# Experts with more than 256 rows: inner rows of three tiles at once instead of two tiles and one more

## The reference, cut to what matters

```python
logits = x @ w_gate                       # 1536 rows, 384 wide, 8 experts
expert_idx = np.argmax(logits, axis=1)
# each expert keeps up to capacity = 384 rows, in order: disp[e]
h = np.maximum(np.einsum('ecd,edf->ecf', disp, w1), 0.0)   # inner rows, 1024 wide
y = np.einsum('ecf,efd->ecd', h, w2)                       # outputs, 384 wide
out[i] = gate_w[i] * y[expert_idx[i], pos[i]]
```

## Time and profile before

| | us |
|---|---|
| median of 3 runs | 458.02 (458.01 to 459.62) |
| the profiled execution | 458.81 |
| its span, first to last instruction | 457.1 |
| VectorE busy | 309.7 (68%) |
| ScalarE busy | 255.3 (56%) |
| GpSimd busy | 57.8 (13%) |

### The profile page before, as it was taken

One profiled execution on the slowest core, in us unless ns is written; L12 is line 12 of the kernel. 1 busy time (PEld: TensorE's weight loads), 2 busy tenths in 40 slices (PEclk: granted clock), 3 DMA queues, 4 the chain that ended last, 5 costly groups with the idle time before them and its releaser, 6 DMA issues.

```text
span 457.1 us, 14532 instructions
## 1 busy us (share of the span) xinstructions
PE 431.2 (94%) x5882; PEld 409.5 (90%) x5882; DVE 309.7 (68%) x763; ACT 255.3 (56%) x527; POOL 57.8 (13%) x78
## 2 busy tenths in 40 slices
PE   2789999999999999999999999999999999999994
PEld 2678899999999999999999999998997789999994
DVE  4787966757686769677867737558556877678510
ACT  2164866456645654565545566575448876686421
POOL 7300000000000100001000200221020333321201
PEclk9999999999999999999999999999999999999998
DMA  8717795880130015001000157431966998610001
GB/s 275 274 60 238 261 325 183 284 329 4 49 145 4 2 44 185 3 1 39 3 1 3 40 209 275 142 120 27 315 215 208 313 353 275 206 61 0 32 1 44
DMA packets 35642, 63.39 MB, mean 139 GB/s; under 512 B 3980, under 2 KB 21950, under 8 KB 35568
## 3 DMA queue, kind: packets, MB, share of 16 engines
q1 hardware_dynamic: 33264, 57.88, 37.3%
q0 software_dynamic: 2304, 4.47, 2.6%
HBM read 50.77 MB, written 14.19 MB: 142 GB/s over the span
## 4 chain that ended last, share of the span: by engine, by line
PE 82%; DVE 6%; issue 5%; ACT 2%; DMA 2%; POOL 1%; POOLq 0%; SPq 0%; DVEq 0%; ACTq 0%
PE bank L718 21%; PE bank L704 19%; PE pair L625 6%; PE bank L931 6%; PE bank L884 5%; PE pair L586 3%; PE pair L884 3%; PE pair L899 3%; PE bank L938 3%; PE bank L899 3%; DVE AD L1224 2%; PE pair L644 2%; DVE KS L1215 2%; DMA stage<-in_moe_w_in 2%; PE pair L679 1%
## 5 line engine op out<-in xcount | busy, mean ns | idle before, releaser
L704 PE MATMUL bank<-XH,W 128*128 128x256 f32 x576 | 118.6, 283 | 0.9 <-ACT RB L1073 0.9
L718 PE MATMUL bank<-W,GH 128*128 128x384 f32 x372 | 98.4, 345 | 0.0
L704 PEld LDWEIGHTS bank<-XH,W 128*128 128x128 f32 x576 | 94.9, 189 | 1.9 <-issue 1.2
L704 PE MATMUL bank<-XL,W 128*128 128x256 f32 x288 | 80.6, 280 | 0.0
L718 PEld LDWEIGHTS bank<-W,GH 128*128 128x128 f32 x372 | 61.7, 188 | 1.3
L1073 ACT ACTIVATE RB<-bank 128x256 f32<-128x256 f32 x96 | 36.7, 382 | 46.6 <-PE bank L704 45.9
L718 PE MATMUL bank<-W,GL 128*128 128x384 f32 x186 | 62.6, 337 | 0.0
L1276 DVE TENSOR_TENSOR GL<-GG,GH 128x256 fp32r<-128x256 f32 x96 | 40.6, 423 | 32.0 <-ACT GH L970 31.5
L970 ACT ACTIVATE GH<-GG 128x256 fp32r<-128x256 f32 x96 | 40.1, 418 | 35.9 <-PE bank L718 34.4
L1215 DVE TENSOR_TENSOR KS<-KS 128x512 f32<-128x512 f32 x72 | 50.3, 699 | 8.8 <-PE pair L625 8.8
L704 PEld LDWEIGHTS bank<-XL,W 128*128 128x128 f32 x288 | 54.3, 188 | 0.0
(11 more groups left out here) (165 smaller groups left out, 716.5 us busy)
## 6 DMA issues: line engine op xcount, KB each, us to landing
raw<-in_moe_w SPq DMA_DIRECT2D x23, 768.0 KB, 7.5
stage<-in_moe_w SPq DMA_DIRECT2D x9, 768.0 KB, 8.1
KS<-in_krw SPq DMA_DIRECT2D x12, 512.0 KB, 5.9
slots<-X SPq DMA_DIRECT2D x8, 579.0 KB, 6.6
VV<-in_v SPq DMA_DIRECT2D x12, 288.0 KB, 6.9
KS<-in_krw SPq DMA_DIRECT2D x12, 256.0 KB, 6.1
stage<-in_moe_w_in SPq DMA_DIRECT2D x4, 768.0 KB, 7.0
stage<-in_moe_w_out SPq DMA_DIRECT2D x4, 768.0 KB, 7.2
```

What stands on the lines that cost most here:

```text
L704: last = nc.tensor.matmul(bank[4 + f % 2][:, 0:2 * P], win[wa][:, c, f * P:(f + 1) * P], xa[:, c, :], start=n == 0, stop=n == 3 * KM - 1)
L718: last = nc.tensor.matmul(bank[6 + m][:, 0:DM], ga[(NF * g + f) % G3][:, cols], wout[wa][:, f, :], start=f == 0 and n == 0, stop=f == NF - ...
```

## The change

Experts with more than 256 rows no longer take the small way for their third tile. `hidden2` gets the number of tiles, and the branches choose between a copy of it that moves 384 columns and one that moves 256; both copies stand in the program. ACT's and DVE's counterparts read 384 or 256 columns the same way. The small way stays for experts of up to 128 rows alone. The three semaphores of the third tile go. On PE:

```diff
-            def hidden2(e):
+            def hidden2(e, tiles):
                 if e > 0:
-                    pe.wait_ge(xl2_ready, MT * e + 2)
+                    pe.wait_ge(xl2_ready, MT * e + tiles)
...
-                            last = nc.tensor.matmul(bank[HB[f % 3]][:, 0:2 * P], w1s(e, wa)[:, c, f * P:(f + 1) * P],
-                                                    xa[:, c, 0:2 * P], start=n == 0, stop=n == 3 * KM - 1)
+                            last = nc.tensor.matmul(bank[HB[f % 3]][:, 0:tiles * P], w1s(e, wa)[:, c, f * P:(f + 1) * P],
+                                                    xa[:, c, 0:tiles * P], start=n == 0, stop=n == 3 * KM - 1)
...
             for e in range(NE):
                 rows = pe.value_load(count_u[0:1, e:e + 1])
                 with pe.If(rows <= P):
-                    hidden_small(e, 0, h2_done)
-                    pe.sem_inc(h3_done, NFE)
+                    hidden_small(e)
                 with pe.Else():
-                    hidden2(e)
                     with pe.If(rows > 2 * P):
-                        hidden_small(e, 2, h3_done)
+                        hidden2(e, MT)
                     with pe.Else():
-                        rows_in(e + 1, 0)
-                        pe.sem_inc(hs_done, 2)
-                        pe.sem_inc(h3_done, NFE)
+                        hidden2(e, 2)
+                    rows_in(e + 1, 0)
+                    pe.sem_inc(hs_done, 2)
                 rows_in(e + 1, 1)
                 outputs2(e, 0)
```

`outputs2` loses its waits on hh3_ready and hl3_ready. On ACT (DVE is alike, with `hidden_low`):

```diff
-            def hidden_high(e):
+            def hidden_high(e, tiles):
                 for f in range(NFE):
                     act.wait_ge(h2_done, NFE * e + f + 1)
-                    nc.scalar.activation(HH[:, f, 0:2 * P], bank[HB[f % 3]][:, 0:2 * P], ACT.Relu).then_inc(hh_ready, 1)
+                    nc.scalar.activation(HH[:, f, 0:tiles * P], bank[HB[f % 3]][:, 0:tiles * P],
+                                         ACT.Relu).then_inc(hh_ready, 1)
...
                 with act.Else():
-                    hidden_high(e)
                     with act.If(rows > 2 * P):
-                        hidden_high_small(e, 2, h3_done, hh3_ready)
+                        hidden_high(e, MT)
                     with act.Else():
-                        act.sem_inc(rh_ready, 2)
-                        act.sem_inc(hh3_ready, NFE)
+                        hidden_high(e, 2)
+                    act.sem_inc(rh_ready, 2)
```

More of the change, by code:

```diff
@@ L146, in rwkv_moe_kernel @@
         SB = (5, 2)
-        SMALL = {0: (2, 4), 2: (7, 3)}
+        SMALL = (2, 4)
         XB = (0, 1, 4)
@@ L898, in hidden_small @@
                         for wa, xa in ((0, XH2), (0, XL2), (1, XH2)):
-                            last = nc.tensor.matmul(bank[SMALL[m][c]][:, 0:CF], xa[:, k_, m * P:(m + 1) * P],
+                            last = nc.tensor.matmul(bank[SMALL[c]][:, 0:CF], xa[:, k_, 0:P],
                                                     w1s(e, wa)[:, k_, c * CF:(c + 1) * CF],
@@ L907, in hidden_small @@
                     pe.wait_ge(rh_ready, 2 * e + c + 1)
-                    if m == MT - 1:
-                        pe.wait_ge(hl_ready, NFE * (e + 1))
                     for f in range(NFE // 2):
@@ L912, in hidden_small @@
                                                    RH[:, c * NFE // 2 + f, :], ident[:, :])
-                    last.then_inc(done, NFE // 2)
+                    last.then_inc(h2_done, NFE // 2)
             def outputs2(e, m):
@@ L1108, in _, with hidden_high_small @@
                 first_rows_high(q)
-            def hidden_high(e):
+            def hidden_high(e, tiles):
                 for f in range(NFE):
                     act.wait_ge(h2_done, NFE * e + f + 1)
-                    nc.scalar.activation(HH[:, f, 0:2 * P], bank[HB[f % 3]][:, 0:2 * P], ACT.Relu).then_inc(hh_ready, 1)
+                    nc.scalar.activation(HH[:, f, 0:tiles * P], bank[HB[f % 3]][:, 0:tiles * P],
+                                         ACT.Relu).then_inc(hh_ready, 1)
                     if f == 2 and e > 0:
                         split_high_expert(e, CH - 1)
-            def hidden_high_small(e, m, done, ready):
-                if m == 0 and e > 0:
+            def hidden_high_small(e):
+                if e > 0:
                     split_high_expert(e, CH - 1)
@@ L1123, in hidden_high_small @@
                     copy(RH[:, c * NFE // 2:(c + 1) * NFE // 2, :],
-                         bank[SMALL[m][c]][:, 0:CF].rearrange("p (f n) -> p f n", n=P)).then_inc(rh_ready, 1)
+                         bank[SMALL[c]][:, 0:CF].rearrange("p (f n) -> p f n", n=P)).then_inc(rh_ready, 1)
                 for c in range(2):
-                    act.wait_ge(done, NFE * e + (c + 1) * NFE // 2)
-                    nc.scalar.activation(HH[:, c * NFE // 2:(c + 1) * NFE // 2, m * P:(m + 1) * P],
+                    act.wait_ge(h2_done, NFE * e + (c + 1) * NFE // 2)
+                    nc.scalar.activation(HH[:, c * NFE // 2:(c + 1) * NFE // 2, 0:P],
                                          bank[SB[c]][:, :].rearrange("p (f n) -> p f n", n=P),
-                                         ACT.Relu).then_inc(ready, NFE // 2)
+                                         ACT.Relu).then_inc(hh_ready, NFE // 2)
             def weighted(e, m):
@@ L1502, in hidden_low, with hidden_low_small @@
                         split_low_expert(e, CH - 1)
[L1504 to L1507, removed]
+            def hidden_low_small(e):
+                for x in (CH - 2, CH - 1):
+                    split_low_expert(e, x)
                 for c in range(2):
-                    dve.wait_ge(high, NFE * e + (c + 1) * NFE // 2)
+                    dve.wait_ge(hh_ready, NFE * e + (c + 1) * NFE // 2)
                     fs = slice(c * NFE // 2, (c + 1) * NFE // 2)
-                    nc.vector.scalar_tensor_tensor(out=HL[:, fs, m * P:(m + 1) * P],
+                    nc.vector.scalar_tensor_tensor(out=HL[:, fs, 0:P],
                                                    in0=bank[SB[c]][:, :].rearrange("p (f n) -> p f n", n=P), scalar=0.0,
-                                                   in1=HH[:, fs, m * P:(m + 1) * P].bitcast(F32), op0=ALU.max,
-                                                   op1=ALU.subtract).then_inc(ready, NFE // 2)
+                                                   in1=HH[:, fs, 0:P].bitcast(F32), op0=ALU.max,
+                                                   op1=ALU.subtract).then_inc(hl_ready, NFE // 2)
             for e in range(NE):
```

26 lines of the change are left out of this document (9 added, 17 removed).

## The result

The changed kernel takes **460.6 us** (median of 20 runs, 457.87 to 463.35) against 458.49 for the kernel before on the same chip: ratio 1.0048, 95% interval 1.0029 to 1.0067. It is slower, as predicted, but by 2.1 us and not by 7.1. Its profiled execution took 460.7 us, with a span of 459.0 us.

What follows compares the result with a forecast made beforehand. TensorE (PE), busy 431.2 of 457.1 us, was taken as the bound. Code waits of +9.9 and PE's work of -2.8 gave +7.1, from the 458.02 median to 465.1 us; range 457.5 to 470.

Steps and rivals of the forecast that it cites:

- PE's own work: Experts 0 and 7: third tile's small way removed, wider matmuls added; -1.4 us each, -2.8 together.
- Evictions cost nothing: ScalarE and DVE reading 384 columns at once is covered by PE's work: cost 0; rival that they bind: 457.2, chance 0.04.
- waits for code: PE waiting for 256-instruction program blocks after taken branches: sum of code +9.9 us; forecast of slower by code, chance 0.62.
- Expert 3: Its jump to block 48 adds +1.0 us, and L956 (later L947) into block 49 adds +0.8.
- Expert 6: Its 256-column code lies in block 54, right behind the jump into block 53: +1.6 us.
- expert 1's skip: Jump from block 42 to 44 over block 43, the only one asked for: +5.3 us; alone passes the 2.8 deciding the sign.
- its clock: Expert 1's pause of 5 us drops PE's granted clock to 0.50: +1.0 us, between nothing and 3.5.
- entering a block asks for the next one: Rule for PE's program blocks, only two held; a block takes 3.7 us idle and about 6 us busy.
- Expert 2: Jump from block 45 to 46 +0.3 us; block 47 asked for at the join, pause 0.7 for 1.71, -1.0.
- Expert 4: 256-column code starts 16 instructions ahead of block 50: wait of 1.8 to 4.1 us, taken as +2.0.
- The rival of blocks at the idle price: Experts' stage leaves DMA freer, so blocks arrive at the idle price: +2.9 less 2.8, 458.1 us; chance 0.12.

Runs made afterwards that it cites:

- the pair without branches: Kernel before and changed kernel, each with arms chosen at build time from this input's counts: 454.06 us (ratio 0.9911) and 452.34 (0.9861).
- The padded kernel before: Kernel before with 82 never-executed PE instruction slots added per expert, giving the changed kernel's 544: 460.22 us, ratio 1.0034.
- the branchless one: Changed kernel with its arms chosen at build time from this input's counts, without branches: 452.34 us, ratio 0.9861.
- moved 40 ahead: Changed kernel with PAGE_PAD 128 for 160, so expert 1's jump stands 40 instructions ahead of block 43: 472.29 us, ratio 1.0294.
- moved 72 ahead: Changed kernel with PAGE_PAD 96 and a never-taken branch in expert 1; its jump stands 72 ahead of block 43: 467.38 us, ratio 1.0194.
- four other layouts of the changed kernel's arms: Changed kernel with copies swapped at PAGE_PAD 128 and 224 (466.43, 459.36 us), and with small path last at 160 and 112 (466.81, 463.75).
- PAGE_PAD 128: 128 instead of 160 semaphore increments on PE ahead of the experts: changed kernel 472.29 us, changed kernel with swapped copies 466.43.
- the kernel with 24: Changed kernel with PAGE_PAD 144 for 160, so expert 1's jump stands 24 instructions ahead of block 43: 461.91 us, ratio 1.0065.
- swapped: Changed kernel with the 256-column copy of hidden2 ahead of the 384-column one: 457.0 us, ratio 0.9960.

## Why the prediction was right and wrong

**Right: PE's own work.** The 384-column rows took 12.50 us for 72 matmuls in expert 7 (427.96 to 440.46), against 8.64 and 5.38 of small way: -1.52, predicted -1.4; in all -1.57 and -1.60 where -1.4 and -1.4 were said. Evictions cost nothing in the experts' stage, as argued; the pair without branches shows it.

**Right: waits for code, not the change's computation, decide the sign.** The padded kernel before has them without the change, the branchless one hasn't them with it. Expert 3: +1.8 predicted, +1.48 measured, but not from where it was to come: the jump that was to add 1.0 took 0.38 us (at 368.2) without a pause, and L947, put at +0.8, gave 1.66 (a pause of 2.34 for 0.68), so the total is in part luck. Expert 6: +1.6 predicted, 1.31 of pause ahead of its first matmul (it stands under expert 5 in the table). The sign is luck in part too. The forecast said that expert 1's skip alone decides it; without that term and its clock its sum is +0.8, which the forecast would have called no difference. The time rose because the terms of experts 2 and 4 were put too small.

**Wrong: expert 1.** The step that failed is "jumps from 10,996 (block 42) to 11,303, in block 44, over block 43, the only one asked for", with +5.3, and +1.0 for the clock behind it. Measured: a jump of 0.39 us, no pause, a clock of 1.00; expert 1 gained the 1.28 that the vanished pause gives (predicted -1.1). That is 6.5 of the difference between +7.1 and what came. The rule "entering a block asks for the next one" was read off packets with a tolerance that I did not write down: where the sequencer runs straight on, a request 50 instructions early or one at the bound makes no stall and so no visible difference in the kernel before. Here the jump stood 8 ahead of the bound, where just that decides, and I gave the rule's exact bound no chance of its own. The price was right: moved 40 ahead, the same jump costs a pause of 4.95 and 1.5 of clock, and moved 72 ahead 4.97 and 1.8, for the +5.3 and +1.0 of the sum. What the Trainium skill says ("Runtime: NRT & Kernel Launch", section Instruction fetch mechanics), a forced fetch at a taken branch outside the two-page window, agrees with 5.43 us at 40 and with 0.39 at 8 only if the window has moved on ahead of the jump.

**Mis-sized: experts 2 and 4.** Expert 2: -0.7 predicted (+0.3 - 1.0), +0.81 measured. Block 47 came 0.4 later than the sum said (asked for at the join, usable at 362.1 against 361.7), PE ran out 0.2 earlier than counted (at 360.8 against 361.0), and its first matmul came 1.0 after the branch ended, behind the count load and two waits, so the pause is 2.37 and not 0.7. Expert 4: +2.0 predicted, +3.72 measured. Its pause of 1.34 was smaller; the 2.4 of clock, lost at the end of the pause ahead of it, was not in the sum, which had put its only clock term at expert 1. (The skip target of L956 is 540 behind the count load and not 537, by the 12,016 above; no bound lies between.)

**The terms together**: -6.5 in expert 1, +1.5 in expert 2, -0.3 in expert 3, +1.7 in expert 4, -0.2 in expert 6, -0.4 in PE's work, against the forecast of +7.1 for the stage: +2.9, and the trace has +2.96. The medians' 2.1 are nearer to the span's 1.9. The rival of blocks at the idle price gave 458.1 and so came nearer than the forecast, but by terms that did not come true either (expert 1 +1.9, expert 2 -1.7, expert 3 -0.7).

**What stays open.** Why the reading ahead did not help expert 2 with PAGE_PAD 128, what decides whether a pause of 2 us costs the clock, and how near to a block's end a target must be to need the next one (3, 12 and 19 do). So which places are good ones was found by running them: four other layouts of the changed kernel's arms were slower than 457.0.

## What to carry to other kernels

In a kernel whose engine is 94% busy and whose program runs over blocks of code, count where each taken jump and its target fall, and treat every distance under some 60 instructions from a bound as unknown: there give both outcomes a chance in the forecast. Before blaming or crediting an edit, run the old kernel padded to the new one's length, and the new one with its branches resolved beforehand; the two together split "work" from "place". And order the arms of an If so that the ones taken often are not reached by a jump over a large copy: that alone gained 3.6 us here (460.6 to 457.0), and 5.9 at PAGE_PAD 128 (472.29 to 466.43).

## What was not expected of the hardware

- Moving the same code by 32 instructions (PAGE_PAD 128 for 160) took the ratio from 1.0048 to 1.0294, some 11 us: more than the whole change under study. By 16 it made 1.0065, no difference that the intervals tell. In the trace with 128 the span is 8.2 us longer; it is of the quickest of the five runs (468.96, granted clock 0.987), and the other four took 471.86 to 472.76 at 0.979 to 0.983. Some 6.5 us more at half the clock, by these shares, is 3.3 us of work lost, an estimate that meets the difference of 468.96 to the median.
- A jump to a place 19 instructions short of a block's end took 6.15 us, though its own block was held.
- The length of a pause of some 2 us does not say whether the clock is lost. It was at 0.50 at the end of the pause of 2.34 (changed kernel, ahead of expert 4) and within 1.0 us behind those of 2.28 (swapped) and 2.19 (padded). It stayed at 1.00 behind 2.37 (changed kernel, ahead of expert 3), and, in the kernel with 24, through pauses of 2.17 and 2.71 with 1.7 us of work between. The rows (PE busy, clock) of the changed kernel around expert 3's start, then of the kernel with 24 from 379.7:

```profile
360.00:363.00 3.00, 0.76 (x5) 1.00 1.05 377
363.00:366.00 3.00, 2.86 (x13) 1.00 1.06 374
```

```profile
379.70:382.40 2.70, 0.04 (x1) 1.00 0.91 287
382.40:386.40 4.00, 4.00 (x34) 1.00 0.35 123
```
